# Transposes of an attention step, issued as blocks or one at a time between big matmuls

## What is computed

```python
# attention, per batch (4), head (8), token t (768), head size 48
f = 1 / (1 + exp(-f_logit))
state = f[t] * state + outer(k[t], v[t])
y[t] = q[t] @ state
# first MLP, d_ff 1536
xn = x / sqrt(mean(x * x) + 1e-6) * rms_g
x = (silu(xn @ w_gate) * (xn @ w_val)) @ w_out
# second MLP, d_ff 2048
h = x @ w_in
g = where(h >= 1, h, where(h <= -1, 0, (h + 1)**2 / 4))
out = g @ w_out
```

## Time and profile before

| | |
|---|---|
| median of 3 runs | 1015.99 us (1015.89 to 1016.22) |
| profiled execution, first to last instruction | 1013.9 us |
| between the two | 2.1 us |
| TensorE busy | 1000.9 us, 99% |
| VectorE busy | 586.5 us, 58% |
| ScalarE busy | 342.7 us, 34% |

### The profile page before, as it was taken

The page is one execution under the profiler, slowest core; times in us unless marked ns, Lnnn a source line. Parts: engine busy times, 40 slices in busy tenths (PEclk is TensorE's granted clock), DMA queues, the critical chain, the costliest instruction groups (busy, mean ns, idle before and its releaser), DMA issues.

```text
span 1013.9 us, 16822 instructions
## 1 busy us (share of the span) xinstructions
PE 1000.9 (99%) x6307; PEld 985.1 (97%) x6307; DVE 586.5 (58%) x1196; ACT 342.7 (34%) x624; POOL 19.5 (2%) x58
## 2 busy tenths in 40 slices
PE   7999999999999999999999999999999999999998
PEld 7899999999999999999999999999999999999998
DVE  8777564665565664664663665545554545454553
ACT  2343322322322322222222444344344443434343
POOL 0000000000000000000000000000000000000000
PEclk9999999999999999999999999999999999999999
DMA  5541111111111011111121230000000000000000
GB/s 187 185 143 40 40 39 41 39 39 47 31 46 39 31 47 39 39 39 39 39 68 48 80 92 2 1 23 0 23 0 23 0 23 0 23 0 23 0 24 24
DMA packets 15768, 42.22 MB, mean 42 GB/s; under 512 B 1408, under 2 KB 8064, under 8 KB 15744
## 3 DMA queue, kind: packets, MB, share of 16 engines
q1 hardware_dynamic: 15744, 41.88, 12.3%
HBM read 37.16 MB, written 4.72 MB: 41 GB/s over the span
## 4 chain that ended last, share of the span: by engine, by line
PE 93%; DVE 4%; issue 1%; POOL 1%; ACT 0%; DMA 0%; POOLq 0%; DVEq 0%
PE gate_ps L399 14%; PE val_ps L399 14%; PE acc L475 13%; PE gate_ps L463 10%; PE val_ps L463 10%; PE acc L421 9%; PE acc L479 7%; PE acc L425 5%; PE y_ps L338 4%; PE tb L313 2%; PE y_ps L334 2%; PE tb L322 2%; DVE qd L717 1%; PE ta L299 1%; DVE kd L726 1%
## 5 line engine op out<-in xcount | busy, mean ns | idle before, releaser
L833 DVE TENSOR_TENSOR h_lo<-h_buf,h_hi 128x384 fp32r<-128x384 f32 x224 | 123.2, 550 | 13.2 <-ACT h_hi L644 6.2
L475 PE MATMUL acc<-h_hi,w_hi 128*128 128x384 f32 x381 | 127.5, 335 | 0.0
L475 PE MATMUL acc<-h_hi,w_lo 128*128 128x384 f32 x381 | 127.3, 334 | 0.0
L637 ACT ACTIVATE act_buf<-act_buf,half_col 128x384 f32<-128x384 f32 x128 | 78.7, 615 | 140.4 <-DVE act_buf L883 140.4
L580 ACT ACTIVATE act_buf<-gate_ps 128x384 f32<-128x384 f32 x96 | 47.2, 491 | 180.9 <-PE gate_ps L399 180.9
L399 PE MATMUL gate_ps<-x_hi,w_hi 128*128 (+1 forms) x288 | 100.5, 349 | 2.0 <-DVE h_buf L822 1.5
L585 ACT ACTIVATE h_hi<-h_buf 128x384 fp32r<-128x384 f32 x96 | 50.4, 525 | 151.0 <-DVE h_buf L828 151.0
L421 PE MATMUL acc<-h_hi,w_hi 128*128 128x384 f32 x288 | 100.4, 349 | 0.0
L399 PE MATMUL val_ps<-x_hi,w_hi 128*128 (+1 forms) x288 | 100.2, 348 | 0.0
L399 PE MATMUL gate_ps<-x_hi,w_lo 128*128 (+1 forms) x288 | 96.7, 336 | 0.0
L421 PE MATMUL acc<-h_hi,w_lo 128*128 128x384 f32 x288 | 96.6, 335 | 0.0
(11 more groups left out here) (117 smaller groups left out, 2040.5 us busy)
## 6 DMA issues: line engine op xcount, KB each, us to landing
raw<-qkf_dram SPq DMA_DIRECT2D x21, 768.0 KB, 4.3
x<-wb_dram SPq DMA_DIRECT2D x12, 576.0 KB, 5.9
v_sb<-v_dram SPq DMA_DIRECT2D x24, 192.0 KB, 2.8
out_dram<-x SPq DMA_DIRECT2D x7, 576.0 KB, 2.8
raw<-wc_dram SPq DMA_DIRECT2D x7, 384.0 KB, 3.1
x<-qkf_dram SPq DMA_DIRECT2D x2, 768.0 KB, 6.5
kd<-wc_dram SPq DMA_DIRECT2D x3, 384.0 KB, 3.2
qd<-wc_dram SPq DMA_DIRECT2D x3, 384.0 KB, 3.4
```

The source lines that it names most:

```text
L475: pe.matmul(acc[:, m, 0:N], wc_part(w, j, 1, m), h_hi[:, j % 2, :], start=(j == 0 and w is w_hi), stop=False)
L637: nc.scalar.activation(act_buf[:, j % 2, :], act_buf[:, j % 2, :], ACT.Square, bias=half_col[:, :], scale=0.5).then_inc(square_ready, 1)
L833: nc.vector.tensor_tensor(h_lo[:, j % 2, :], h_buf[:, j % 2, :], h_hi[:, j % 2, :].bitcast(F32), ALU.subtract).then_inc(done, 1)
```

## The change

`turn_kd` and `turn_x` issue one transpose for each call instead of all four or three; the waits stand ahead of the first, the signal behind the last. In the stages they are no longer called by `attention` at their slot but by a new function `between`, which the projection that follows this slot calls after each of its matmuls (m counts them): after matmuls 0, 2, 4 and 6 for keys, 0, 2 and 4 for rows. Slot 3j is handed to value j, 3j+1 to project_out j-1, 3j+2 to gate j+1. In the prologue the transposes are issued as before.

```diff
-                def turn_kd(n, c):
-                    pe.wait_ge(kd_ready, n + 1)
-                    if not isinstance(n, int) or n > 0:
-                        pe.wait_ge(scores_ready, 2 * n)
-                    for p in range(NP):
-                        mm = pe.transpose(ta[:, p * PR:(p + 1) * PR], kd[0:PR, c % 2, p, :], ident[0:PR, 0:PR])
-                    mm.then_inc(kdT_made, 1)
+                def turn_kd(n, c, p):
+                    if p == 0:
+                        pe.wait_ge(kd_ready, n + 1)
+                        if not isinstance(n, int) or n > 0:
+                            pe.wait_ge(scores_ready, 2 * n)
+                    mm = pe.transpose(ta[:, p * PR:(p + 1) * PR], kd[0:PR, c % 2, p, :], ident[0:PR, 0:PR])
+                    if p == NP - 1:
+                        mm.then_inc(kdT_made, 1)
...
+                def turn_x(n, k, bank=tb):
+                    if k == 0:
+                        pe.wait_ge(xs_ready, n + 1)
+                        pe.wait_ge(state_ready, n + 1)
+                    mm = pe.transpose(bank[:, k * P:(k + 1) * P], xs[:, k * P:(k + 1) * P], ident[:, :])
+                    if k == KM - 1:
+                        mm.then_inc(xT_made, 1)
...
-                        if o == 4:
-                            turn_kd(n, c)
-                        elif o == 6:
+                        if o == 6:
                             score(n, c)
...
-                        elif o == 13:
-                            turn_x(n)
+
+                def between(i, slot, m):
+
+                    if i is None or m % 2:
+                        return
+                    for c in range(CT):
+                        n = i * CT + c
+                        o = slot - WINDOW * c
+                        if o == 4 and m // 2 < NP:
+                            turn_kd(n, c, m // 2)
+                        elif o == 13 and m // 2 < KM:
+                            turn_x(n, m // 2)
...
-                def project(i, j, part, bank):
+                def project(i, j, part, bank, following, slot):
...
+                            if k < KM - 1 or t < 2:
+                                between(following, slot, 3 * k + t)
...
                     for m in range(KM):
-                        for w in (w_hi, w_lo):
+                        for t, w in enumerate((w_hi, w_lo)):
                             pe.matmul(acc[:, m, 0:N], wb_part(w, j, 2, m), h_hi[:, j % 2, :],
                                       start=(j == 0 and w is w_hi), stop=False)
+                            between(following, slot, 2 * m + t)
                     pe.wait_ge(h_lo_ready, i * JB + j + 1)
                     for m in range(KM):
                         mm = pe.matmul(acc[:, m, 0:N], wb_part(w_hi, j, 2, m), h_lo[:, j % 2, :],
                                        start=False, stop=(j == JB - 1))
+                        if m < KM - 1:
+                            between(following, slot, 2 * KM + m)
...
-                            gate(i, j)
+                            gate(i, j, following, 3 * j - 1)
                         if following is not None:
                             attention(following, 3 * j)
-                        value(i, j)
+                        value(i, j, following, 3 * j)
                         if following is not None:
                             attention(following, 3 * j + 1)
                         if j > 0:
-                            project_out(i, j - 1)
+                            project_out(i, j - 1, following, 3 * j + 1)
```

More of the change, by code:

```diff
@@ L376, in first_attention @@
                     keep_warm(WARM_START)
-                    turn_kd(0, 0)
+                    for p in range(NP):
+                        turn_kd(0, 0, p)
                     score(0, 0, True)
@@ L383, in first_attention @@
                         if n + 1 < CT:
-                            turn_kd(n + 1, n + 1)
+                            for p in range(NP):
+                                turn_kd(n + 1, n + 1, p)
                         attend(n, n, 1)
@@ L390, in first_attention @@
                             keep_warm(WARM_LAST)
-                        turn_x(n, (gate_ps, val_ps)[n % 2])
+                        for k in range(KM):
+                            turn_x(n, k, (gate_ps, val_ps)[n % 2])
                         keep_warm(WARM_ROWS)
-                def project(i, j, part, bank):
+                def project(i, j, part, bank, following, slot):
                     par = i % 2
                     for k in range(KM):
-                        for w, x in ((w_hi, x_hi), (w_hi, x_lo), (w_lo, x_hi)):
+                        for t, (w, x) in enumerate(((w_hi, x_hi), (w_hi, x_lo), (w_lo, x_hi))):
                             mm = pe.matmul(bank[:, 0:N], wb_part(w, j, part, k), x[:, par, k, :],
@@ L401, in project, with gate @@
                                            stop=(k == KM - 1 and w is w_lo))
+                            if k < KM - 1 or t < 2:
+                                between(following, slot, 3 * k + t)
                     return mm
-                def gate(i, j):
+                def gate(i, j, following=None, slot=0):
                     pe.wait_ge(w_lo_ready, j + 1)
@@ L408, in gate, with value, project_out @@
                     pe.wait_ge(gate_used, i * JB + j + 1)
-                    project(i, j, 0, gate_ps).then_inc(gate_made, 1)
-                def value(i, j):
+                    project(i, j, 0, gate_ps, following, slot).then_inc(gate_made, 1)
+                def value(i, j, following, slot):
                     pe.wait_ge(h_ready, i * JB + j + 1)
-                    project(i, j, 1, val_ps).then_inc(val_made, 1)
-                def project_out(i, j):
+                    project(i, j, 1, val_ps, following, slot).then_inc(val_made, 1)
+                def project_out(i, j, following=None, slot=0):
                     pe.wait_ge(h_hi_ready, i * JB + j + 1)
```

## The result

The changed kernel takes 1021.68 us, median of four runs (1020.51 to 1022.86), against 1015.97: a ratio of 1.0055, 95% interval 1.0043 to 1.0067, so it is slower by 5.7 us. The four lie in two pairs, 1020.5 and 1020.7 on one side and 1022.7 and 1022.9 on the other, and the kernel before has such longer runs too (up to 1020.0 in 22 later ones), so the median holds about 1 us that is not the change's, and by the lower pair the change costs 4.5 to 4.7 us. The profiled execution took 1020.71 us; its span is 4.9 us longer than before. Forecast were +3.9 us and the range 1017.6 to 1022.4.

What follows compares the result with a forecast made beforehand. TensorE, busy 99% of the span, was taken as the bound. 126 transposes at 0.118 (keys) or 0.113 us (rows), less 10.7 us for blocks, gave +3.85; 1015.99+3.85 = 1019.8, with slow starts 1019.9, range 1017.6 to 1022.4.

Steps and rivals of the forecast that it cites:

- the lost cover at gate 8: Gate 8, rows of chunk 1: three transposes, free inside the wait for gate_used 7, now stand behind it; 2.4 us.
- the keys of chunk 0 at h_lo: Output projection of block 0: the fourth key transpose now stands behind the wait for h_lo; 0.8 us in all.
- counts of 13 and 8 waits: Waits read from the profile: 13 of the gates for VectorE's product (L822), 8 of L425 for h_lo.
- (0.49-0.27)/2: Pace of transposes inside a block of rows, taken as 0.108 us, the lowest price of a lone transpose.
- low bound: Whole change with a lone transpose at 0.108 us: +2.9 us, time 1018.9.
- t for keys: Price of one lone key transpose between big matmuls: about 0.118 us, high bound 0.14.
- t for rows: Price of one lone row transpose between big matmuls: 0.113 us.
- keys, chunk 1: nothing waits there: Gate 5: no wait covers the block, so each stage pays four lone transposes less the block's 0.43 us.
- Late consumers at nothing: Copies and VectorE work behind the later transposes delay no matmul, cost nothing; value 11 is tightest.
- forecast slack of 0.3 us: Behind value 11: VectorE's pair ends at about 257.25, the next gate wants it at 257.56.
- Rival C: Slower still: slow starts after every key transpose (0.14 us each, time 1021.2) or an overrun in value 11 (1021.3); chance 0.17.
- Rival B: No change: a lone transpose costs between 0.069 and 0.101 us, for instance 0.095, +1.3 us, time 1017.3; chance 0.09.

## Why the prediction was right, and where its sizes were off

**Direction and mechanism.** A transpose between big matmuls costs one exposed load, as it does in a block; this held on every timeline and in the experiment with 256 columns. Of the 4.69 us in the stages, 2.3 are the lost cover at gate 8 (forecast 2.4; 2.33 came back when that block was put back, and 2.44 of the change's cost vanished when the wait was taken away), and 0.82 the keys of chunk 0 at h_lo (0.123 a stage in stages 1 to 6, 0.08 in stage 0; forecast 0.8; it fell to about 0.04 a stage when the wait was taken away). Two readings of the prediction were off without a part in the sum. Its counts of 13 and 8 waits add matmuls and weight loads; gate 8 waits once a stage. And (0.49-0.27)/2 is 0.11 and not 0.108, so its low bound should read +3.2 and not +2.9.

**t for keys** was set at 0.118. Measured in gate 5 and value 8 it is (0.43+0.06)/4 = 0.1225, 0.25 us over 14 groups. **t for rows** was 0.113; with 0.011 over the block for chunk 0 and 0.048 for chunk 2 it is 0.115 and 0.128, 0.36 us over 14 groups. Some 0.03 of the extra of the last is a run of slow starts (0.177, 0.185, 0.176, 0.182) behind the third transpose. In the kernel before such a run follows every block of keys but few blocks of rows (4 of 21), so here it is new, and the prediction had priced it for keys alone.

**A cover was missed.** The step "keys, chunk 1: nothing waits there" holds for six stages. In stage 0 gate 5 waits, and by the times the same mechanism as at gate 8 costs 0.33 instead of 0.06. I had read the places in the middle stages alone.

**Late consumers at nothing** was right. The tightest chain, ScalarE's rounding and VectorE's two instructions behind value 11, against the gate that needs them (rows of after, to be held against the earlier trace rows):

```profile
257.90 0.49 ACT L571 ACTIVATE x_hi<-tb 128x384 f32 x1 [0.82 <-PE tb L347]
...
258.54 0.56 DVE L803 TENSOR_TENSOR x_lo<-tb,x_hi 128x384 f32 x1 [3.29 <-ACT x_hi L571]
259.01 0.55 DVE L840 TENSOR_TENSOR h_buf<-gate_ps,act_buf 128x384 f32<-128x384 f32 x1
...
259.86 0.34 PE L412 MATMUL gate_ps<-x_hi,w_hi 128*128 x1
```

VectorE is done at 259.56 and the gate starts on time at 259.86: the forecast slack of 0.3 us is there.

**Rival C**, slow starts after each key transpose, has a grain of truth: pairs between them run at 0.172 to 0.180, but the run of 0.178, 0.185, 0.176, 0.182 comes once, after the last. So t is 0.1225 and not 0.14. **Rival B** falls with the measured t.

**The time.** 1015.99+3.85 was meant for an ordinary execution. The two shorter runs lie at 1020.5 and 1020.7, 0.6 to 0.8 us above 1019.9. The spans differ by 4.9 us instead of 3.85: 0.25 and 0.36 are the sizes of t, 0.27 the missed cover, and 0.2 lies outside the stages. The median of 1021.68 lies another 1 us up for a reason that the prediction does not have.

## What to carry to other kernels

In this kernel, where every matmul has a load of its own, a short one between long ones is paid at the load of the one behind it, so spreading short ones hides nothing; twice the columns came at the same price. Before moving a block past a wait, look whether the wait is what pays for it, in every stage and not only in a typical one: here 0.33 us of transposes a stage were free under a late VectorE result. Such a wait is itself the thing to attack: two changes of order on VectorE, which is busy 58% of the time, gave 4.6 us where the change on TensorE lost 4.7.

## What the hardware showed that I had not expected

TensorE's clock can fall to 0.50, the lower level of 1.2 GHz, in the prologue. Five of the fourteen profiles show it. The first gate starts at 37.2 to 37.8 us in the nine others, at 39.6 and 39.7 in two of the five and at 41.1 to 41.4 in three, so the fall costs 2 or 4 us, as much as the change under test. One of the longer falls, in the profile of the run with chunk 1's rows as a block; busy time by engine, clock third from the end:

```profile
13.00:16.00 3.00, 2.55 (x19) 2.45 (x19) 2.96 (x7) 0.00 (x0) 0.00 (x0) 0.87 0.06 25
16.00:20.00 4.00, 4.00 (x21) 3.91 (x22) 1.75 (x6) 0.76 (x2) 0.00 (x0) 0.50 0.02 4
20.00:24.00 4.00, 4.00 (x27) 3.78 (x26) 3.90 (x11) 0.36 (x2) 0.78 (x2) 0.50 0.55 199
24.00:28.00 4.00, 4.00 (x33) 4.00 (x33) 1.87 (x5) 1.54 (x2) 0.00 (x0) 0.82 0.00 0
```

In the three us in which it fell the engine was idle for 0.45 us. That alone does not decide it. The profile of the changed kernel above has 0.49 us of idle time there and keeps the full clock:

```profile
13.00:16.00 3.00, 2.51 (x22) 2.41 (x23) 2.96 (x7) 0.00 (x0) 0.00 (x0) 1.00 0.12 48
```

What decides whether a run has the fall stays open.

Transposes can be followed by a run of slow starts of the big ones (0.178, 0.185, 0.176, 0.182 us instead of 0.173, 0.03 us in all). Neither their number nor their kind decides it. In the kernel before, the run follows all 21 blocks of four keys and 4 of the 21 blocks of three rows. In both kernels with blocks and changes on VectorE alone, where TensorE's order is the same, it follows none of the 21 blocks of keys and all 21 of rows. In the changed kernel it follows the last lone transpose of keys wherever enough big ones come behind (21 of 21). Behind the added blocks of four in the second MLP it comes 128 times of 128, which makes the price of one there 0.116 instead of 0.110. Why is open, and so a block's price in these traces is known to 0.03 us only.
